# An expert's output product as phases of seven products, its weights prepared beside the attention

## The reference

```python
p_packed = sm_attn(p, k, v)               # 8 batches, 8 heads, 32 packs, 576 keys, 64 dims
out = sm_attn(q, p_packed, p_packed)      # the 576 tokens of q attend the 32 packs
x = out.transpose(0, 2, 1, 3).reshape(4608, 512)
xn = x / sqrt(mean(x * x) + 1e-6) * rms_g
x = (silu(xn @ w_gate) * (xn @ w_val)) @ w_out      # first expert, hidden size 1536
h = x @ w_in                                        # second expert, hidden size 2048
return (max(h, 0) + alpha * min(h, 0)) @ w_out2
```

## Time and profile before

| | |
|---|---|
| median of 3 runs | 1443.06 us (1441.87 to 1443.1) |
| the profiled execution | 1442.03 us |
| its span | 1440.2 us |
| TensorE, VectorE, ScalarE, GpSimd busy | 99%, 67%, 50%, 22% |
| tiles of A and attention | 0 to 736.7 us |
| second expert, five rounds | 736.7 us to the end |

### The profile page before, as it was taken

How to read it: one execution, slowest core, us unless ns; L and a number is a source line. 1 busy time by engine, 2 the same in 40 slices (tenths; PEclk the granted TensorE clock), 3 DMA queues, 4 the chain that set the end, 5 groups by cost and what they waited for, 6 DMA issues and landing times.

```text
span 1440.2 us, 24192 instructions
## 1 busy us (share of the span) xinstructions
PE 1429.2 (99%) x9334; PEld 1230.1 (85%) x9334; DVE 958.0 (67%) x1530; ACT 716.1 (50%) x1174; POOL 316.9 (22%) x543
## 2 busy tenths in 40 slices
PE   8999999999999999999999999999999999999998
PEld 4988878888887888889888888888888888889998
DVE  6775756647575664742337885788678857886786
ACT  4454454445445444532235653565456545654564
POOL 2803545243454424443800000000000000000000
PEclk9999999999999999999999999999999999999999
DMA  9414586866868687347237867777777777768775
GB/s 359 142 42 139 157 285 187 237 224 176 271 168 265 187 235 231 98 136 246 88 116 253 287 230 237 254 278 246 230 259 279 240 241 249 256 232 261 253 265 187
DMA packets 174770, 314.16 MB, mean 218 GB/s; under 512 B 22208, under 2 KB 128704, under 8 KB 160192
## 3 DMA queue, kind: packets, MB, share of 16 engines
q1 hardware_dynamic: 174512, 312.56, 67.1%
q10 hardware_dynamic: 144, 0.07, 0.0%
HBM read 250.19 MB, written 54.92 MB: 212 GB/s over the span
## 4 chain that ended last, share of the span: by engine, by line
PE 97%; DVE 1%; ACT 0%; DMA 0%; issue 0%; SPq 0%; DVEq 0%; ACTq 0%
PE psum L924 31%; PE psum L926 30%; PE psum L925 30%; PE psum L1122 3%; PE psum L1023 1%; PE psum L947 1%; PE psum L996 1%; DMA k_sb<-k_t 0%; PE psum L1052 0%; PE psum L1051 0%; PE psum L1055 0%; PE psum L981 0%; DVE g_sb L1990 0%; PE psum L961 0%; PE psum L1087 0%
## 5 line engine op out<-in xcount | busy, mean ns | idle before, releaser
L924 PE MATMUL psum<-an_hi,m_hi 128*128 128x288 f32 x768 | 232.4, 303 | 1.2 <-DVE an_lo L1830 1.2
L925 PE MATMUL psum<-an_hi,m_lo 128*128 128x288 f32 x768 | 225.9, 294 | 0.0
L926 PE MATMUL psum<-an_lo,m_hi 128*128 128x288 f32 x768 | 225.7, 294 | 0.0
L924 PE MATMUL psum<-stage_hi,ring 128*128 128x480 f32 (+1 forms) x560 | 206.9, 369 | 0.1
L926 PE MATMUL psum<-stage_lo,ring 128*128 128x480 f32 (+1 forms) x560 | 206.8, 369 | 0.0
L925 PE MATMUL psum<-stage_hi,ring 128*128 128x480 f32 (+1 forms) x560 | 206.8, 369 | 0.0
L924 PE MATMUL psum<-x_hi,ring 128*128 128x480 f32 (+1 forms) x560 | 206.8, 369 | 0.0
L926 PE MATMUL psum<-x_lo,ring 128*128 128x480 f32 (+1 forms) x560 | 206.8, 369 | 0.0
L925 PE MATMUL psum<-x_hi,ring 128*128 128x480 f32 (+1 forms) x560 | 206.8, 369 | 0.0
L1562 ACT CAST stage_hi<-g_sb 128x480 fp32r<-128x480 f32 (+1 forms) x240 | 138.0, 578 | 121.6 <-PE psum L926 121.6
L2002 DVE TENSOR_TENSOR stage_lo<-g_sb,stage_hi 128x480 fp32r<-128x480 f32 (+1 forms) x240 | 150.1, 634 | 49.3 <-ACT stage_hi L1562 48.9
(11 more groups left out here) (183 smaller groups left out, 2443.6 us busy)
## 6 DMA issues: line engine op xcount, KB each, us to landing
ring<-w_down SPq DMA_DIRECT2D x70, 1024.0 KB, 5.3
ring<-w_up SPq DMA_DIRECT2D x40, 1024.0 KB, 5.3
gv_sb<-w_gv SPq DMA_DIRECT2D x39, 1024.0 KB, 5.9
ring<-w_up SPq DMA_DIRECT2D x40, 768.0 KB, 4.5
k_sb<-k_t SPq DMA_DIRECT2D x16, 576.0 KB, 5.2
q_sb<-q_t SPq DMA_DIRECT2D x8, 1152.0 KB, 5.6
w_up<-parts_hi SPq DMA_DIRECT2D x16, 448.0 KB, 6.4
w_up<-parts_lo SPq DMA_DIRECT2D x16, 448.0 KB, 6.1
```

The source lines that it names most:

```text
L924: nc.tensor.matmul(dst, w_hi, hi, start=start, stop=False, skip_group_check=onto)
L925: nc.tensor.matmul(dst, w_lo, hi, start=False, stop=False, skip_group_check=onto)
L926: return nc.tensor.matmul(dst, w_hi, lo, start=False, stop=stop, skip_group_check=onto)
```

## The change

Tiles of A keep their 24 blocks and lose everything behind the hidden block: no `h_hi`/`h_lo`, no `down`, no copies of y, no `w_out` split, no rest tile. The hidden block is stored whole to a new buffer in memory, `h_mid`. With banks 4 to 7 free, gate and value alternate between two pairs of banks (from block 7 of tile 0 on). `gv_sb` stays in place for all batches. `scaled` and `normed` move from GpSimd to VectorE. The attention of a batch is spread over two tiles: scores, maximum, exponential and `turn_keys` of batch c + 1 stand one tile earlier (`NEXT`; for batch 2 `NEXT_BUT_ONE`, in tile 0), the last two folds are carried into the next tile.

The first expert's output becomes five "out" phases of the kind of `down2`: seven products, six duos, 252 matmuls each, at `WIDTHS` 464 four times and 448, with data read back from `h_mid` and split by ScalarE and VectorE. `w_out` gets the same seven combinations: 12 more parts, so 44, in the numbers 5, 6, 6, 6, 6, 6, 6, 3 per tile, the first three of them loaded at block 12 of tile 0. The order of phases is `PHASES`. The second expert's first data come from the out phase's buffers by DMA and are changed and split by VectorE and ScalarE beside the second out phase.

```diff
-TILE = 512
...
-GV_SLOTS = 3
-SLOTS, WIDE_SLOTS, FIRST_ACTS = 3, 2, 4
-LAG, WIDE_LAG = 2, 3
+ACTS = 6
+SINGLE = 6
...
+    "DVE": {("after", 0): ["norm0", "norm1", "packed"], ("after", 2): ["scaled"],
+            ("after", 3): ["turn_s0", "gram"], ("after", 4): ["max2_0", "shift0"],
...
+NEXT = {
+    "PE": {("ready", 9): ["scores0_ready"], ("after", 9): ["scores0", "scores1_ready", "scores1"]},
+    "DVE": {("between", 11): ["max0"], ("between", 13): ["max1"], ("between", 15): ["turn_keys"]},
+    "Activation": {("between", 9): ["scores0", "scores1"], ("between", 13): ["exp0", "exp1", "silu"]},
+}
...
-PART_PLACES = {b: ([5 * (b - 1), 5 * (b - 1) + 1], [5 * (b - 1) + n for n in range(2, 5)]) for b in range(1, BATCH)}
-PART_PLACES[BATCH - 1] = (PART_PLACES[BATCH - 1][0], [])
-assert sum(len(n) for two in PART_PLACES.values() for n in two) == PARTS
-WIDTHS = [480, 480, 480, 480, 384]
+PARTS_OF = [5, 6, 6, 6, 6, 6, 6, 3]
+PART_PLACES = [{} for b in range(BATCH)]
+for b, count in enumerate(PARTS_OF):
+    PART_PLACES[b] = {(13 + 2 * n if b == 0 else 1 + 4 * n): sum(PARTS_OF[:b]) + n for n in range(count)}
+assert sorted(n for places in PART_PLACES for n in places.values()) == list(range(PARTS))
...
-WIDTHS = [480, 480, 480, 480, 384]
+PARTS_OF = [5, 6, 6, 6, 6, 6, 6, 3]
...
+PHASES = [("out", 0), ("out", 1), ("up", 0), ("down", 0)]
+for t in range(1, ROUNDS):
+    PHASES += ([("out", t + 1)] if t + 1 < ROUNDS else []) + [("up", t), ("down", t)]
...
+ROLE = ["b11", "b12", "b12", "t3", "b21", "b22", "b12"]
...
+        def pair_of_banks(n):
+            return 0 if n < SINGLE or n % 2 == 0 else 4
+
...
-                sp.wait_ge(newton_step, 3 * c + 3)
-                sp.wait_ge(y_stored, 32 * (c - 1))
+                sp.wait_ge(pp_mm, 2 * c)
                 sp.wait_ge(rows_out, 16 * GROUPS * (c - 1))
...
+            def store_hidden(b, i):
+                src, n = act_of(b, i)
+                slot, f = n % ACTS, i % NF1 if b == 0 else i // 2
                 sp.wait_ge(h32_done, BLOCKS_OF * b + i + 1)
...
+                at, width = SEQ * b, SEQ
+                if b == 0:
+                    at, width = i // NF1 * HALF, HALF
+                sp.dma_start(h_mid[:, f, at:at + width], act_sb[:, slot, 0:width]).then_inc(h_out[slot], 16)
...
+            def load_hidden(k, role):
+                t = WIDE[k][1]
+                rows, cols = int(role[1]) - 1, int(role[2]) - 1
+                at = STARTS[t] + cols * WIDTHS[t]
+                sp.dma_start(block_of(k, role, slice(0, DUOS1)), h_mid[:, rows::2, at:at + WIDTHS[t]]).then_inc(h_in[role], 16)
...
+            def move_parts(b, i):
+                if b == 0 and i == 12:
+                    sp.wait_ge(an_lo_done, 2)
                     for n in range(PART_SLOTS):
                         load_part(n)
...
+                n = PART_PLACES[b].get(i)
+                if n is not None:
+                    store_part(n)
+                    if 0 < n < PARTS - PART_SLOTS + 1:
+                        load_part(n + PART_SLOTS - 1)
...
-            for c in range(1, BATCH + 1):
-                early, late = PART_PLACES.get(c - 1, ([], []))
-                for n in early:
-                    combine(n)
-                if c < BATCH:
-                    scaled(c)
-                for n in late:
-                    combine(n)
-                if c < BATCH:
-                    normed(c, 0)
-                    normed(c, 1)
-
...
+            for n in range(PARTS):
+                combine(n)
...
+                n = BLOCKS_OF * b + i
+                for part, dst in ((0, gate_ps(n)), (1, val_ps(n))):
+                    reached(pe, silu_done if part == 0 else h32_done, block_before(n))
...
-                for i in range(BLOCKS_OF + WIDE_LAG):
-                    if i < BLOCKS_OF:
-                        up_block(b, i, i // 2, i % 2, at)
-                    for piece in OUT_PIECES.get(i, []):
...
+            def scaled(c):
+                dve.wait_ge(ppt_copied, c + 1)
+                reached(dve, m_mm, NF1 // 2 * (c - 1))
+                nc.vector.tensor_tensor(pp_tg[c % 2][:], ppt_ps.rearrange("p (q k) -> p q k", q=PAIRS),
+                                        g_sb[:].unsqueeze(2).to_broadcast([P, PAIRS, PACK]), ALU.mult).then_inc(ppg_done, 1)
+
+            def normed(c, h):
+                dve.wait_ge(newton_step, 6 + 3 * c)
+                nc.vector.tensor_tensor(a2[:, h], a2[:, h], rinv[:, h, :].unsqueeze(1).to_broadcast([P, GROUPS, HALF]),
+                                        ALU.mult).then_inc(a2n_done, 1)
...
+            def wide(k, p, ups):
+
+                w, depth, dst = width_of(k), DEPTH[k], pair_ps(k, p, width_of(k))
+                pair_free(k, p, ups)
+                for begin, end in WIDE_PARTS[WIDE[k][0]]:
+                    weights = next_page()
                     for j in range(begin, end):
-                        u = UNITS * t + DUOS * p + j
+                        u = UNIT_AT[k] + depth * p + j
                         pe.wait_ge(stage_lo_done, u + 1)
                         for side in range(2):
                             mm = three_passes(dst[:, side, :], weights[:, j - begin, side, 0, :],
                                               weights[:, j - begin, side, 1, :], stage_hi[:, u % STAGES, 0:w],
                                               stage_lo[:, u % STAGES, 0:w], j == 0 and p not in DOWN_ONTO,
-                                              j == DUOS - 1, p in DOWN_ONTO)
+                                              j == depth - 1, p in DOWN_ONTO)
...
+            def change_first_x(n):
+                w = WIDTHS[0]
+                to, of, less = ((3, 5, 2), (2, 2, 0), (1, 5, 2), (6, 4, 1))[n]
+                for name in "rhef":
+                    dve.wait_ge(first_x_in[name], 16)
+                reached(dve, first_x_changed, n)
+                nc.vector.tensor_tensor(x_raw[:, to, :, 0:w], x_raw[:, of, :, 0:w], x_raw[:, less, :, 0:w],
+                                        ALU.subtract).then_inc(first_x_changed, 1)
```

1399 lines of the change are left out of this document (622 added, 777 removed), and 12 rows, old and new, of tables (DVE_FIRST, LATER, SECOND).

## The result

| | before | changed |
|---|---|---|
| median | 1442.91 us | 1462.95 us (1458.8 to 1472.1) |
| ratio to before | | 1.0147, 95% interval 1.0106 to 1.0188 |
| profiled execution, span | 1440.2 us | 1470.3 us |
| TensorE busy | 99% | 96% |

What follows compares the result with a forecast made beforehand. TensorE, busy 99% of the span, was taken as the bound: 1440.2 − 35.0 + 15.5 + 1 + 12.5 + 2.5 + .4 = 1437.1 us span, 1438.9 device, 1439.5 us forecast; range 1426 to 1454.

Steps and rivals of the forecast that it cites:

- TensorE's work, −35.0 us: Whole kernel: matmuls removed save 297.0 us, five new output phases add 262.0 us, net −35.0 us.
- Moved or hidden: Tiles: VectorE's work falls to 43.0 us, 82% of a 52.4 us tile, so hidden; about the same traffic in less time.
- Stall 1: Start of tile 1: packed of batch 2 waits for the keys behind the fourth part in SyncE's queue; +15.5 us, bounds 12 and 18.
- The walk: Start of tile 1: steps from the first part loads at 59.7 us to packed at about 104, against TensorE ready at 88.5.
- The sign named for it: Start of tile 1: packed near 104 us with 13 to 17 us of idle before it, released by the keys' transfer.
- "+1 us" for the clock: Head of tile 1: TensorE's clock drops after its long idle wait there; +1 us, bounds 0 and 4.
- Stall 2: Tiles 1 to 5: a later batch's exponential delays VectorE's sums for means; 2.5 us a tile, +12.5, bounds 5 and 20.
- Stall 3: Second output phase: VectorE also makes the second expert's first data, 51 to 56 us against 52.8; +2.5, bounds 0 and 10.
- VectorE and GpSimd do block each other: Rival, tiles: VectorE, slowed by GpSimd, grows by 13.7 us and becomes the bound; 1453 us, chance .18.
- Transfers as a bound of the phases: Rival, output phases: if only 290 GB/s lasts, five phases grow by 2.8 us each; 1453 us, chance .14.
- A slower kernel: Whole kernel: a time over 1446 us, chance .33, mostly from VectorE, the transfers and the forecast's high end.

Runs made afterwards that it cites:

- e18_all_behind_k: e17 with the part stores of tiles 1 to 5 at blocks 5, 8, 12, 15, 19, 22, all behind the k load; 1436.6 us.
- e2: Changed kernel with the values' load issued behind the k load (block 8 instead of 2; in tile 0 block 12 instead of 8); 1463.4 us.
- e1: Changed kernel with the keys of batch 2 sent at block 19 of tile 0, ahead of the fourth part's store; 1464.6 us.
- e5: Changed kernel with tile 0's part stores two to four at blocks 21 to 23 and the keys of batch 2 at block 19; 1467.7 us.
- e11: e9 plus, in tile 0, keys at block 17 ahead of the third part and batch 1's norm ahead of block 21's product; 1450.6 us.
- e13: e11 with the last tile's first loads spread and the keys of batch 2 stored ahead of q's load in tile 0; 1446.3 us.
- e15: e13 with tile 0's keys stored at block 19, read at 20, q behind, four parts in tile 0 and their stores moved; 1450.1 us.
- e17: e15 with tile 1's part stores behind the k load and parts per tile 4, 6, 6, 6, 6, 6, 7, 3; 1443.7 us.
- e3: Changed kernel with the keys' turn on VectorE moved behind means, block 15 to 17, in tiles 1 to 5; 1459.5 us.
- e9: Changed kernel with, in tiles 1 to 5 only, the values' load behind the k load and the keys' turn behind means; 1451.7 us.
- e4: Changed kernel with GpSimd doing one 128x128 addition per weight part instead of fifteen operations, stored parts zeros; 1450.4 us.
- e14: Changed kernel with only the head's moves of e11 and e13 (keys at block 17 ahead of q, norm ahead of product); 1463.9 us.

## Why the prediction was wrong, point by point

- **TensorE's work, −35.0 us: right.** From the second expert's first product to the end it took 861.9 us; the sum of matmuls at the rows' prices and the end is 860.4 (698.8 + 262.0 − 105.5, and 4.7 + .4). The phases are full. In the tiles TensorE's work is 53.0 us each where 52.4 was forecast (e18_all_behind_k, busy 212.4 of the 220 us from 156 to 376, four tiles, at full clock).
- **"Moved or hidden", VectorE 43.0 us a tile: right** in size (42.5). **The step that failed** stands in the same paragraph: "the store of the hidden blocks comes ...: about the same traffic in less time". Nothing was drawn from it, so how long k takes to land is in no term of the sum. SyncE's transfers ran at 267 GB/s from 168 to 400 us against 222 before. The load of k, 1.15 MB in two halves, landed after 9.6 us in the median, before after 5.2, while TensorE stands before the scores 7.3 to 8.0 us after its issue; so it waited 0.8 to 2.4 us in each of tiles 1 to 5. With the values' load behind it, k lands after 5.5 us and the wait is gone (e2). The second thing left out is what SyncE's queue holds besides the keys: the load of k and the stores that free the six slots stand behind the same waits for GpSimd.
- **Stall 1, +15.5: the path was right, TensorE's side of it and the cure were not.** The walk (104 us) was 6 us short of the measured 110.45: the first load left at 66.0 us in place of 59.7, since tile 0 has waits of its own (a part took 7.2 us, as forecast). The sign named for it was 13 to 17 us of idle before packed; measured were 5.8. TensorE came late itself, at 104.65 us where the walk had 88.5: it had waited 2.7 and 0.9 us for a fold's low part (92.3 and 100.8 us) and ran at a granted clock of 0.50 from 95.0. More waits lie under the one for the keys. e1, e5, e11 and e13 each take away one that is then last, and packed comes 0.5 to 6.7 us earlier; only e15, which takes the wait of SyncE from before the hidden stores too, gets 9.4, and the gain stays only when (e17, e18) SyncE waits for GpSimd before no transfer that is needed soon.
- **"+1 us" for the clock, bounds 0 and 4: mis-sized.** It cost 16.3 us in the profiled execution. The prediction had only the long wait at the head (0.50 from 95 to 115 us). But stretches of 3.4 us at 0.50 also came in tile 2 behind the k wait of 2.4 us, in tiles 3, 4 and 5 behind the wait before means of 1.7 to 1.8 us, and in tile 6 behind one of 1.7 us. The same wait before means in tiles 1 and 2 (at 151.3 and 210.2 us) was followed by none, so its length alone does not tell. The Trainium skill (TensorE: Matmul & The Clock Gate, Part 1: The HAM clock gate) states the fall after idling, and the trace agrees; the rule was in the prediction, but applied in one place. In e18, with waits of at most 1.4 us behind tile 0, there is no such stretch from 103 to 1429 us.
- **Stall 2, +12.5: mechanism right, but under a third of what a tile loses.** The wait before means was 1.7 to 1.8 us a tile (forecast 2.1 to 2.5), and e3 and e9 show that it depends on the keys' turn. The period was 58.4 in place of 54.9 and of the 52.4 without a stall: in tiles 2 to 5 means took 1.8 us on average, the wait for k 1.8 and the lower clock 1.7. That e9 then runs at just the forecast's 54.9 is chance: the wait before means is at most 1.0 us there, and other short waits make up the rest.
- **Stall 3, +2.5: 6.9.** Not VectorE beside the second phase, which was full at 38.2 of 40 us, but the last tile's slots: SyncE issues three loads of 1392 KB and four of 768 KB from 472.1 to 488.7 us, a hidden store behind them takes 12.0 us to land, a silu waits 7.65 us for its slot, and TensorE, after 3.7 us of idle at 502.4, runs at a granted clock of 0.50 until about 508.
- **The rivals.** VectorE and GpSimd do block each other, but VectorE's work grows by 1 us a tile, not by 13.7. Transfers as a bound of the phases: no; the phases never waited for a page. Transfers late in the tiles, that rival's true place, were not priced. A slower kernel had a chance of .33, but from VectorE and from the phases, not from this.

**What stays open.** e4 shows 12.6 us for GpSimd's work, of which e18 regains the queue's share; how much of the rest is VectorE's slower operations was not separated. The scatter of the changed kernels (up to 14.5 us between executions, up to 3 us for the kernel before) has no shown cause: the changed kernel's slowest execution has its lowest mean clock (.984), but the slowest of e11 (1459.4 us at .996) and of e17 (1450.0 at .998) have the highest of theirs. What starts a low stretch behind one wait and not behind an equal one was not tried.

## What to carry to other kernels

A queue that is issued in order is a resource with a critical path of its own: for each wait in it, list what stands behind, not only what it is for, and put waits for a slow producer behind the loads that the next stage needs. When a stage gets a third shorter at the same traffic, price the landing time of every transfer in it against the new slack. And where a wait is cured and the time stays, look for the next one in the same queue before giving up the theory: here single moves of order (e1, e2, e3, e5, e14) changed the median by something between 3.5 us less and 5 us more, none clear of the scatter, and all together gave 26.

## What the runs showed of the hardware

- In tiles 1 to 5, idle stretches of 1.7 to 2.4 us in an otherwise full stream were followed by 3.4 us at a granted clock of 0.50 in four of six cases (from 190.5, 269.0, 327.1 and 385.1 us), some 1.7 us lost each. At this clock matmuls of 288 columns start 0.24 us apart in place of 0.13 (113 to 115 and 193 us against 116 and 194). The kernel before has no such stretch in its tiles.
- SyncE's issue of a transfer took longer in the changed kernel: the second half of a part's load 0.49 us in the median before and 1.26 after, the first half 4.0 us at the longest, against 1.5. So the issuer itself is delayed, too; that the number of transfers in flight does it was not tested.

```profile
91.29 4.03 SPq L625 DMA_DIRECT2D parts_raw<-w_parts  x1
98.63 1.12 SPq L625 DMA_DIRECT2D parts_raw<-w_parts  x1
99.80 1.29 SPq L626 DMA_DIRECT2D parts_raw<-w_parts  x1
101.13 1.01 SPq L594 DMA_DIRECT2D a_mid<-a_rows  x2
```

- Among VectorE's operations of 0.4 us and more, GpSimd slowed only some with two inputs in SBUF, by 5 to 32% in the mean (the low part of the sums 588 ns against 446, that of the probabilities 797 against 753); others with two such inputs, as L1574 (752 and 752), kept their time.
- The keys' store of 288 KB landed after 2.4 us in the median of the changed kernel, and after 8.7 in e11_norm_first in tile 0, behind a load of 1.15 MB that was issued just ahead; ahead of that load (e13_keys_before_q) it took 5.6 at most.
